# TensorE's g_lo products placed between the first products of a later chunk

## The reference

```python
w = exp(weight_gen - max over the 7 taps); w = w / (sum + 1e-9)
mixed[b, s, h*24+g] = sum over k of w[b, s, h, k] * x_pad[b, s + k, h*24+g]   # 7-tap window ending at s
h = mixed @ w_in                                  # (16384, 192) @ (192, 2048)
g = where(h > 0, h, exp(min(h, 0)) - 1)           # ELU
out = g @ w_out                                   # (16384, 2048) @ (2048, 192)
```

## Time and profile before

| | |
|---|---|
| Time, median of 3 runs | 1227.78 us (1226.43 to 1228.07) |
| The profiled execution's own time | 1226.57 us |
| Its span | 1224.8 us |
| TensorE products busy | 97% |
| TensorE weight loads busy | 88% |
| VectorE, ScalarE, POOL busy | 64%, 78%, 64% |
| Mean granted TensorE clock | 0.994 of 2.4 GHz |

### The profile page before, as it was taken

The page is one execution under the profiler, slowest core; times in us unless marked ns, Lnnn a source line. Parts: engine busy times, 40 slices in busy tenths (PEclk is TensorE's granted clock), DMA queues, the critical chain, the costliest instruction groups (busy, mean ns, idle before and its releaser), DMA issues.

```text
span 1224.8 us, 19582 instructions
## 1 busy us (share of the span) xinstructions
PE 1184.6 (97%) x6662; PEld 1072.9 (88%) x6662; DVE 787.3 (64%) x1298; ACT 954.7 (78%) x1773; POOL 783.3 (64%) x360
## 2 busy tenths in 40 slices
PE   2799999999999999999999999999999999999998
PEld 1688999999999999999999999999999999999998
DVE  7956666666666666666666666666666666666655
ACT  3577888787888787888787888787888787888786
POOL 8676566776656776566776656776566776666700
PEclk9899999999999999999999999999999999999999
DMA  7211222211222211222211222211222211221100
GB/s 230 63 49 31 80 80 79 73 55 31 79 79 79 74 53 30 79 79 79 72 56 30 79 79 79 74 51 33 79 79 79 74 53 31 79 79 43 37 20 14
DMA packets 52301, 80.27 MB, mean 66 GB/s; under 512 B 5416, under 2 KB 35492, under 8 KB 52256
## 3 DMA queue, kind: packets, MB, share of 16 engines
q1 hardware_dynamic: 52256, 79.82, 21.2%
HBM read 55.03 MB, written 24.77 MB: 65 GB/s over the span
## 4 chain that ended last, share of the span: by engine, by line
PE 92%; POOL 4%; issue 2%; DVE 1%; DMA 0%; SPq 0%; POOLq 0%; ACT 0%; DVEq 0%
PE slot L648 47%; PE acc L654 28%; PE acc L658 17%; POOL prod L362 2%; POOL prod L366 1%; DVE prod L520 0%; POOL prod L369 0%; DVE prod L524 0%; POOL win_rest_lo L338 0%; POOL prod L370 0%; DMA xwin<-in_x_dram 0%; SPq L259 0%; POOL wsum L342 0%; DVE prod L528 0%; POOL probs L332 0%
## 5 line engine op out<-in xcount | busy, mean ns | idle before, releaser
L602 DVE SCALAR_TENSOR_TENSOR slot<-em,slot 128x512 f32<-128x512 f32 x512 | 356.4, 696 | 407.0 <-ACT em L479 401.8
L654 PE MATMUL acc<-wout,g_hi 128*128 128x384 f32 x2048 | 463.2, 339 | 9.2 <-DVE g_lo L608 9.2
L476 ACT ACTIVATE em<-slot 128x512 f32<-128x512 f32 x512 | 305.2, 596 | 191.5 <-PE slot L648 191.3
L654 PEld LDWEIGHTS acc<-wout,g_hi 128*128 128x128 f32 x2048 | 374.2, 188 | 51.6 <-issue 9.5
L608 DVE TENSOR_TENSOR g_lo<-slot,g_hi 128x512 fp32r<-128x512 f32 x511 | 349.1, 683 | 0.0
L479 ACT ACTIVATE em<-em 128x512 f32<-128x512 f32 x512 | 323.4, 632 | 16.3
L658 PE MATMUL acc<-wout,g_lo 128*128 128x192 f32 x2048 | 327.2, 267 | 4.0 <-DVE g_lo L608 4.0
L658 PEld LDWEIGHTS acc<-wout,g_lo 128*128 128x128 f32 x2048 | 312.1, 190 | 7.0 <-DVE g_lo L608 4.6
L362 POOL TENSOR_TENSOR prod<-xwin,probs 128x5376 f32<-128x5376 f32 (+1 forms) x32 | 308.4, 9638 | 8.4 <-POOL xt L391 6.6
L485 ACT ACTIVATE g_hi<-slot 128x512 fp32r<-128x512 f32 x511 | 297.3, 582 | 16.4 <-DVE slot L602 16.4
L648 PE MATMUL slot<-xt,win_hi 128*128 128x512 f32 x512 | 215.1, 420 | 2.7 <-DVE xt L565 2.7
(11 more groups left out here) (54 smaller groups left out, 550.1 us busy)
## 6 DMA issues: line engine op xcount, KB each, us to landing
xwin<-in_x_dram SPq DMA_DIRECT2D x30, 960.0 KB, 5.0
out_dram<-outs SPq DMA_DIRECT2D x32, 384.0 KB, 2.4
turned_dram<-turned SPq DMA_DIRECT2D x124, 96.0 KB, 2.0
x_main<-turned_dram SPq DMA_DIRECT2D x31, 256.0 KB, 2.8
x_rest<-turned_dram SPq DMA_DIRECT2D x62, 128.0 KB, 3.0
wg<-in_weight_gen_dram SPq DMA_DIRECT2D x32, 112.0 KB, 2.2
wout_raw<-in_moe_w_out_dram SPq DMA_DIRECT2D x4, 384.0 KB, 9.3
win_raw<-in_moe_w_in_dram SPq DMA_DIRECT2D x1, 768.0 KB, 6.4
```

What stands on the lines that cost most here:

```text
L476: nc.scalar.activation(em[:, i % 2, :], slot[s][:], ACT.Exp).then_inc(s_exp, 1)
L602: nc.vector.scalar_tensor_tensor(out=slot[s][:], in0=em[:, i % 2, :], scalar=0.0, in1=slot[s][:], op0=ALU.min, op1=ALU.max).then_inc(s_g, 1)
L654: pe.matmul(acc[j][:, 0:2 * d_model], g_hi[:, f % GBUFS, chunk(j)], wout[:, f, :], start=(f == 0), stop=False)
```

## The change

`first_product` gets an argument `between`, a function that it calls behind each of its first four products. In chunks 1 to 14 round f now begins with the four g_hi products of chunk f, behind their wait for s_ghi; then come the first products of chunk f + 3 with one g_lo product of chunk f behind each of the first four. The wait for s_split stands between the first of the first products and the first g_lo product, and s_used is incremented by the fourth g_lo product. In the last block, where there is no chunk f + 3 left, the four g_lo products follow the g_hi products directly. Chunks 0 and 15 keep their order (`edge_product` behind the first products). The first block's wait for a part of wout moves ahead of the first products.

```diff
--- before.py
+++ after.py
@@ -638,7 +638,7 @@
                 last = pe.transpose(slot[s][:, W:W + P], rest, ident[:])
                 last.then_inc(s_filled, 1)
 
-            def first_product(parity, f, s):
+            def first_product(parity, f, s, between=None):
 
                 cols = chunk(f)
                 for k, (w, v) in enumerate((
@@ -646,38 +646,29 @@
                         (win_hi[:, cols], xt_lo[:, parity, :]), (win_rest_hi[:, cols], xt[:, parity, 1, :]),
                         (win_rest_lo[:, cols], xt[:, parity, 1, :]))):
                     last = pe.matmul(slot[s][:], w, v, start=(k == 0), stop=(k == 4))
+                    if between and k < TILES:
+                        between(k)
                 last.then_inc(s_filled, 1)
 
-            def second_product(b, f):
-
-                def hi(j):
-                    pe.matmul(acc[j][:, 0:2 * d_model], g_hi[:, f % GBUFS, chunk(j)], wout[:, f, :],
-                              start=(f == 0), stop=False)
-
-                def lo(j):
-                    return pe.matmul(acc[j][:, d_model:2 * d_model], g_lo[:, f % GBUFS, chunk(j)],
-                                     wout[:, f, 0:d_model], start=False, stop=(f == CHUNKS - 1))
-
-                if f in (0, CHUNKS - 1):
-
-                    pe.wait_ge(s_split, b.count(CHUNKS, f + 1))
-                    for j in range(TILES):
-                        if f == 0:
-
-                            ge(pe, s_out, b.count(TILES, j + 1 - TILES))
-                        hi(j)
-                        last = lo(j)
-                        if f == CHUNKS - 1 or j == TILES - 1:
-                            last.then_inc(s_used, 1)
-                else:
-
-                    pe.wait_ge(s_ghi, b.count(CHUNKS, f + 1))
-                    for j in range(TILES):
-                        hi(j)
-                    pe.wait_ge(s_split, b.count(CHUNKS, f + 1))
-                    for j in range(TILES):
-                        last = lo(j)
-                    last.then_inc(s_used, 1)
+            def high_of(b, f, j):
+                pe.matmul(acc[j][:, 0:2 * d_model], g_hi[:, f % GBUFS, chunk(j)], wout[:, f, :],
+                          start=(f == 0), stop=False)
+
+            def low_of(b, f, j):
+                return pe.matmul(acc[j][:, d_model:2 * d_model], g_lo[:, f % GBUFS, chunk(j)],
+                                 wout[:, f, 0:d_model], start=False, stop=(f == CHUNKS - 1))
+
+            def edge_product(b, f):
+
+                pe.wait_ge(s_split, b.count(CHUNKS, f + 1))
+                for j in range(TILES):
+                    if f == 0:
+
+                        ge(pe, s_out, b.count(TILES, j + 1 - TILES))
+                    high_of(b, f, j)
+                    last = low_of(b, f, j)
+                    if f == CHUNKS - 1 or j == TILES - 1:
+                        last.then_inc(s_used, 1)
 
             pe.wait_ge(s_ident, 3)
             pe.wait_ge(s_vmix, VMIX)
@@ -701,23 +692,43 @@
 
                 for f in range(CHUNKS):
                     pos = f + LAG
+                    edge = f in (0, CHUNKS - 1)
+                    if not b.has_previous and f in (p.start for p in WOUT_PARTS):
+
+                        pe.wait_ge(s_wlo, 4 + f // (CHUNKS // 4))
+                    if not edge:
+
+                        pe.wait_ge(s_ghi, b.count(CHUNKS, f + 1))
+                        for j in range(TILES):
+                            high_of(b, f, j)
+
+                    def low_between(j):
+
+                        if j == 0:
+                            pe.wait_ge(s_split, b.count(CHUNKS, f + 1))
+                        last = low_of(b, f, j)
+                        if j == TILES - 1:
+                            last.then_inc(s_used, 1)
+
+                    between = None if edge else low_between
                     if pos < CHUNKS:
                         slot_free(pos)
                         if not b.has_previous and pos == WIN_PARTS[1].start // P:
 
                             pe.wait_ge(s_wlo, 3)
                             pe.wait_ge(s_plo, 1)
-                        first_product(q, pos, slot_of(q, pos))
+                        first_product(q, pos, slot_of(q, pos), between)
                     elif b.has_next:
                         if pos == CHUNKS:
 
                             pe.wait_ge(s_xtlo, b.count(2, 2))
                         slot_free(pos)
-                        first_product(1 - q, pos - CHUNKS, slot_of(q, pos))
-                    if not b.has_previous and f in (p.start for p in WOUT_PARTS):
-
-                        pe.wait_ge(s_wlo, 4 + f // (CHUNKS // 4))
-                    second_product(b, f)
+                        first_product(1 - q, pos - CHUNKS, slot_of(q, pos), between)
+                    elif not edge:
+                        for j in range(TILES):
+                            low_between(j)
+                    if edge:
+                        edge_product(b, f)
 
             all_blocks(pe, body)
```

## The result

The changed kernel takes 1241.32 us (1240.85 to 1242.75, 4 runs) against 1227.68 us (1226.43 to 1228.07, 4 runs): a ratio of 1.0115, 95% interval 1.0097 to 1.0132. It is slower by 13.6 us. Its profiled execution took 1240.87 us, 14.3 more than that of before, with a span of 1239.1. All four executions of the changed kernel show a mean granted clock of 0.990 or 0.991. The 54 executions of the kernel before that ran beside the experiments show 0.993 to 0.996; one more (1660 us, 0.658) was in a slow state and is left out of the comparisons of experiments 2, 10 and 11.

What follows compares the result with a forecast made beforehand. The prediction took TensorE, 97% busy, as the bound. Regrouping 0 plus waits 5.6 + 1.6 + 0.9 + 0.9 + 1.15 = 10.2 us on the profiled 1226.57 gave 1236.7, forecast as 1237 us, range 1229 to 1247.

Steps and rivals of the forecast that it cites:

- a start at the half clock: First block: if the hole keeps the clock down longer, the four first products left over cost 1.7 us, not 0.9.
- w and l in rounds of 0.34 us: Sign of being right: a first product (w) and a g_lo product (l) alternate on TensorE, 0.23 + 0.11 us.
- a round of 2.30: Sign of being right: TensorE's time per steady chunk stays at 2.30 us; 2.20 would show the forecast wrong.
- Regrouping costs nothing: In 14 of a block's 16 chunks, the new order adds 0 to the products; bounds +4 and -47 us.
- The rival that the loads hide: Weight loads of g_lo products or their successors start earlier: -47 us, 1190 us with the waits; chance 0.10.
- Chunk 9: ScalarE's two copies to xt delay g_hi; TensorE waits 0.18 us, 31 times: 5.6 us, ends 0 and 11.5.
- The copies of cross: Block start: ScalarE's four copies delay chunk 1's g_hi; wait 0.05 us, 31 times: 1.6 us, ends 0 and 4.7.
- The start: First block, chunk 1: four first products of chunk 4 are left behind the wait for g_lo: 0.9 us, to 1.7.
- The second block: VectorE's transpose waits for POOL's mix, leaving four first products of chunk 7 behind the hole: 0.9 us, to 1.7.
- The end: The last chunk's w5, its fifth first product, comes later behind chunk 12's g_hi and g_lo products: +1.15 us.
- The rival of a margin that breaks in every chunk: TensorE then runs at the pace of exp, em, g_hi, H: 27 us on top, 1264 us; chance 0.10.
- cross free and chunk 9 halved: Low end of the likeliest case: no wait from the cross copies, half of chunk 9's wait: 1231 us.

Runs made afterwards that it cites:

- experiment 2: Kernel before, with each g_lo product (l) of chunks 1 to 14 cut to 128 columns of 192: 1227.89 us, ratio 1.0005.
- experiment 10: Kernel before, with VectorE's turn and ScalarE's copies to xt in chunks 7 and 12 instead of 4 and 9, except in the first block: 1223.65 us.
- experiment 11: As experiment 10, plus w_out's second split ahead of POOL's product, later quarters in chunks 7 and 10, first block's turn and copies at 9 and 13: 1216.93 us.
- experiment 3: Kernel before, with g_lo products of chunk f - 1 between the first products of chunk f + 3, still ahead of chunk f's g_hi products: 1228.72 us.
- experiment 1: Kernel before, with g_lo products of chunks 1 to 14 widened to 248 columns: two groups, 1226.77 to 1228.17 (3 runs) and 1244.18 to 1245.92 us (6).
- experiment 6: Changed kernel, with a third, unused copy of 128 x 512 on ScalarE in chunk 9: 1257.23 us, ratio 1.0235.

## Why the prediction was right

The way and the places were as forecast, and the size lies in the range (1237, 1229 to 1247, measured 1241.3). It does not lie on the sum: 10.2 us were added up, and the profiled executions differ by 14.3. The range held because it allowed for a start at the half clock. Of the signs named, w and l in rounds of 0.34 us, a round of 2.30, 31 waits in chunk 9 of 0.22 us and a longer end all came.

- **Regrouping costs nothing.** Right: experiment 3 has it alone at +1.2 us (the bound named was +4), and experiment 2, with the lower group of experiment 1, shows the mechanism. The rival that the loads hide (-47 us) is dead. The Trainium skill's rule for it ("TensorE: Matmul & The Clock Gate", section "Back-to-back issue gap", loads and products pipelined through a window of 64) is not borne out here, if it is read as loads drawn ahead of more than one product: in none of the 13 traces does any load start before the product in front of it, and apart from waits and the narrow l of experiment 2 it starts within 0.05 us of that product's start.
- **Chunk 9, 31 x 0.18 = 5.6 us.** Right: 0.187, 5.8 us, and experiment 6 gives the same margin a second time (0.52 added, 0.50 measured).
- **The copies of cross, 31 x 0.05 = 1.6 us.** 0.043 each, 1.3 us.
- **The start, 0.9 us.** The mechanism was right, the size was not. Of block 1's 2.8 us some 0.3 are the terms above, so the start cost 2.5 us. The step priced four w at the full clock. In the trace four w and four l together ran at 0.50 (2.73 us from 47.06 to 49.79, twice what the rate of 1.00 gives). Before, only the four l were left then, and the clock had risen: 0.45 us. That is 2.28 more, and the H behind them are slower until 50.4. The bound of 1.7 for the half clock was too low as well: four w at half the rate are 1.84, and the l among them were left out.
- **The second block, 0.9 us.** It cost 1.7 beyond the terms above between the two profiled executions. Against the traces with the old order and the clock at 0.50 for as long (43.54 to 43.72) it is 0.4 to 0.6. So no run here tells whether 0.9 was too small.
- **The end, 1.15 us.** 1.2.
- **Not in the sum:** about 0.05 us per middle block in rounds of 2.300, 1.5 us. Kernels without any wait and with an l of another width or place have blocks of 36.773 too, so half of it is not particular to this change; why is open.
- **The rival of a margin that breaks in every chunk** did not come: rounds of 2.300 wherever ScalarE has no extra work, so 0.19 us was enough. Its number does not follow from its words: a way of 0.25 instead of 0.16 us would still be inside the margin, and 0.06 on top of it needs a way of 0.41.
- **Smaller slips.** The sum was put on the profiled execution, which lay 1.2 us under the median; on the median it gives 1238.0. With cross free and chunk 9 halved the sum is 1232.3, not 1231. At the half clock four H and a w from 43.25 end near 45.1, not 44.96. None of them changes the outcome.

## What to carry to other kernels

Before reordering products to hide weight loads, look in the trace at what a load's start coincides with; if it is always the product just ahead, a short product costs its successor's load wherever it stands: behind an l, an H or a w alike. Fewer loads might help; no run here tried it. Count the distance from a producer to its consumer in the new order, with everything that slips in between the two, against the worst chunk and not the usual one: here 0.19 us of margin held in 12 of the 14 reordered chunks of a block and failed in chunk 9 and, by 0.04 us, in chunk 1, where ScalarE had copies to make beside. And work that is moved behind a hole at the start is paid twice if TensorE's granted clock is at half then, as in the first block here.

## What the runs showed of the hardware

- A product of 128, 192 or 248 columns, with a weight load of 128 x 128 behind it, costs the same 0.112 to 0.115 us from start to start (experiment 2, the kernel before, the lower group of experiment 1).
- At 248 columns, the time fell into two groups 17 us apart, on one chip within one series; at 128 columns and at 192 it did not.
- VectorE's split of w_out (both inputs in SBUF) took 10.19 us when it started 0.3 us behind POOL's product of 9.70 us, and two of them took 2.14 us when they came first. The Trainium skill says so ("SBUF — State Buffer", section "SBUF: two separate sides": the pair of ports that the two share is locked for a whole instruction and the loser blocks), and the traces agree.
